# Inverse units in three products, and another order of the work within each step

## The reference

```python
def _attn_ref(x, w_r, w_i, b_r, b_i):          # x: 4 x 3008 x 256
    X = np.fft.rfft(x, axis=1)
    Xr, Xi = (X.real.astype(np.float32), X.imag.astype(np.float32))
    Yr = Xr @ w_r - Xi @ w_i + b_r
    Yi = Xr @ w_i + Xi @ w_r + b_i
    lam = 0.01
    Yr = np.sign(Yr) * np.maximum(np.abs(Yr) - lam, 0.0)
    Yi = np.sign(Yi) * np.maximum(np.abs(Yi) - lam, 0.0)
    Y = Yr.astype(np.float64) + 1j * Yi.astype(np.float64)
    return np.fft.irfft(Y, n=x.shape[1], axis=1).astype(np.float32)

def _moe_ref(x, w_in, w_out, alpha):           # 12032 x 256, 256 x 2048, 2048 x 256
    h = x @ w_in
    g = np.maximum(h, 0.0) + alpha * np.minimum(h, 0.0)
    return (g @ w_out).astype(np.float32)
```

## Time and profile before

| | us |
|---|---|
| median of three runs | 1419.74 |
| lowest, highest | 1418.84, 1421.32 |
| the profiled execution, its own time | 1419.24 |
| its span in the profile | 1417.4 |
| busy in it: TensorE, VectorE | 1380.9, 951.3 |
| busy in it: ScalarE, GpSimd | 743.6, 308.7 |

### The profile page before, as it was taken

One profiled execution on the slowest core, in us unless ns is written; L12 is line 12 of the kernel. 1 busy time (PEld: TensorE's weight loads), 2 busy tenths in 40 slices (PEclk: granted clock), 3 DMA queues, 4 the chain that ended last, 5 costly groups with the idle time before them and its releaser, 6 DMA issues. The chain is left out here.

```text
span 1417.4 us, 21513 instructions
## 1 busy us (share of the span) xinstructions
PE 1380.9 (97%) x7012; PEld 1166.2 (82%) x7012; DVE 951.3 (67%) x1826; ACT 743.6 (52%) x1646; POOL 308.7 (22%) x353
## 2 busy tenths in 40 slices
PE   6998999999999999999999999999999999999997
PEld 3987888888888888888888888888888888888886
DVE  5786677877855557877765556787876555555554
ACT  3775555656544445655654445565664444444443
POOL 1433532222201412222211231222220010001000
PEclk9999999999999999999999999999999999999999
DMA  6644522122210431212211232222121011101101
GB/s 223 193 151 133 158 61 74 52 67 64 47 39 25 134 100 53 71 48 75 56 34 39 73 109 69 58 70 63 53 53 37 16 32 26 19 14 32 21 15 15
DMA packets 163166, 94.72 MB, mean 67 GB/s; under 512 B 110424, under 2 KB 140680, under 8 KB 163056
## 3 DMA queue, kind: packets, MB, share of 16 engines
q1 hardware_dynamic: 158250, 88.91, 23.6%
q10 hardware_dynamic: 4806, 4.45, 1.0%
HBM read 55.78 MB, written 37.49 MB: 66 GB/s over the span
## 5 line engine op out<-in xcount | busy, mean ns | idle before, releaser
L1014 DVE SCALAR_TENSOR_TENSOR g_raw<-negpart,keep,h_ps 128x502 f32<-128x502 f32 (+1 forms) x384 | 282.4, 736 | 375.0 <-ACT negpart L790 372.5
L790 ACT ACTIVATE negpart<-h_ps 128x502 f32<-128x502 f32 (+1 forms) x384 | 224.7, 585 | 471.4 <-PE h_ps L464 471.2
L464 PE MATMUL out_ps<-g_hi,wout_hi 128*128 128x502 f32 (+1 forms) x768 | 313.3, 408 | 6.6 <-DVE g_lo L915 4.7
L464 PE MATMUL h_ps<-y_hi,win_hi 128*128 128x502 f32 (+1 forms) x768 | 300.6, 391 | 0.8 <-DVE y_lo L915 0.5
L464 PE MATMUL h_ps<-y_lo,win_hi 128*128 128x502 f32 (+1 forms) x768 | 300.1, 391 | 0.0
L464 PE MATMUL out_ps<-g_hi,wout_lo 128*128 128x502 f32 (+1 forms) x768 | 300.0, 391 | 0.0
L464 PE MATMUL h_ps<-y_hi,win_lo 128*128 128x502 f32 (+1 forms) x768 | 299.5, 390 | 0.0
L464 PE MATMUL out_ps<-g_lo,wout_hi 128*128 128x502 f32 (+1 forms) x768 | 299.0, 389 | 0.0
L915 DVE TENSOR_TENSOR g_lo<-g_raw,g_hi 128x502 fp32r<-128x502 f32 (+1 forms) x384 | 271.3, 707 | 0.1
L799 ACT ACTIVATE g_hi<-g_raw 128x502 fp32r<-128x502 f32 (+1 forms) x384 | 236.0, 615 | 0.3 <-DVE g_raw L1014 0.3
L464 PEld LDWEIGHTS out_ps<-g_hi,wout_hi 128*128 128x128 f32 x768 | 145.0, 189 | 39.5 <-DVE g_lo L915 10.7
(11 more groups left out here) (121 smaller groups left out, 1972.6 us busy)
## 6 DMA issues: line engine op xcount, KB each, us to landing
pair_raw<-fwd_scratch SPq DMA_DIRECT2D x96, 128.0 KB, 2.2
back_raw<-inv_scratch SPq DMA_DIRECT2D x61, 192.0 KB, 2.6
table<-in_twiddles_dram SPq DMA_DIRECT2D x28, 384.0 KB, 3.5
x_raw<-in_x_dram SPq DMA_DIRECT2D x64, 160.0 KB
inv_scratch<-inv_sb SPq DMA_DIRECT2D x36, 256.0 KB, 2.2
fwd_scratch<-staging SPq DMA_DIRECT2D x44, 192.0 KB, 2.1
out_dram<-turned SPq DMA_DIRECT2D x124, 40.0 KB, 2.0
inv_scratch<-inv_sb SPq DMA_DIRECT2D x24, 128.0 KB, 2.6
```

The lines of the kernel that those rows point to most:

```text
L464: mm = pe.matmul(ps, lhs, rhs, start=(first and n == 0), stop=(last and n == len(terms) - 1), **kw)
L790: act.activation(negpart[:, q % 2, 0:size], h_ps[:, q % 2, 0:size], ACT.Relu, scale=-1.0).then_inc(negpart_done, 1)
L1014: dve.scalar_tensor_tensor(g_raw[:, q % 2, 0:size], negpart[:, q % 2, 0:size], keep[:, m:m + 1], h_ps[:, q % 2, 0:size], ALU.mult, ALU.add ...
```

## The change

**Three matmuls.** For the pairs in the loop the load brings the first 32 of the 96 rows a second time into partitions 96 to 127 of `back_raw`, and the remaining 64 rows of each of the two blocks into the two halves of a spare buffer (`inv_sb[:, 2]`): four DMAs where there was one. ScalarE splits all 128 partitions of back_raw and then the 128x256 of the spare buffer (its hi goes for the moment into the second half of back_lo). VectorE, in the new `rest_first`, replaces partitions 96 to 127 of back_hi by the lo parts of those 32 rows. GpSimd makes the lo parts of the remaining rows for both blocks in one 128x256 operation. In `idft_parts` the rows 96 to 127 hold the hi columns of the first 32 rows again, zeros beside them. So back_hi with 188 columns gives hi x hi, hi x lo and a third of lo x hi; one more matmul with the new table `idft_rest` (188 columns: the remaining rows for block 0, then for block 1, zeros between) gives the rest for both blocks. A unit is three matmuls of 188 columns.

**Order in a step.** TensorE: output before inverse1. ScalarE: split_pair and split_back directly behind split_bent, the twiddle split there too and one step earlier, split_y near the end. VectorE: rest_pair and rest_first before shrink, rest_y last. GpSimd: twiddle rest one step earlier. y_part now lies in the buffer of bias.

```diff
         idft_parts = sb("idft_parts", [P, 2, NA], F32R)
+        idft_rest = sb("idft_rest", [P, 2, NA], F32R)
...
         shr_hi, shr_lo = (sb(f"shr_{h}", [P, 2, DIM], F32R) for h in ("hi", "lo"))
         inv_sb = sb("inv_sb", [P, 3, DIM])
 
-        back_raw = sb("back_raw", [ROWS, 2 * DIM])
+        back_raw = sb("back_raw", [P, 2 * DIM])
         back_hi, back_lo = (sb(f"back_{h}", [P, 2, 2 * DIM], F32R) for h in ("hi", "lo"))
...
 
         def back_arrived(eng, v):
             if v < HEAD_V:
                 eng.wait_ge(head_loaded[v], 16 * 6)
             else:
-                eng.wait_ge(back_loaded, 16 * (v - HEAD_V + 1))
+                eng.wait_ge(back_loaded, 64 * (v - HEAD_V + 1))
 
         def out_place(s):
             return s % OUT_HEAD if s < S_EARLY else (s - S_EARLY) % OUT_RING
...
                 if v == HEAD_V:
                     for k in range(3):
                         sp.wait_ge(inv_stored[k], 16 * GROUPS)
@@ -345,6 +351,11 @@
                     sp.wait_ge(couple_stored, 16 * PAIRS // 2 * g)
                 sp.dma_start(back_place(v).rearrange("r (b d) -> r b d", b=2),
                              inv_dram[g, :, b:b + 2, :]).then_inc(back_loaded, 16)
+                sp.dma_start(back_raw[ROWS:P, :].rearrange("r (b d) -> r b d", b=2),
+                             inv_dram[g, 0:P - ROWS, b:b + 2, :]).then_inc(back_loaded, 16)
+                for k in range(2):
+                    sp.dma_start(inv_sb[64 * k:64 * k + 64, 2, :],
+                                 inv_dram[g, P - ROWS:ROWS, b + k, :]).then_inc(back_loaded, 16)
 
             def load_head(v):
 
...
             def inverse1(u):
                 v, h = divmod(u, 2)
                 pe.wait_ge(back_lo_done, v + 1)
+                if v >= HEAD_V:
+                    pe.wait_ge(back_part_done, v - HEAD_V + 1)
                 if u == 0:
...
+                if u >= I_HEAD:
+                    for b in range(2):
+                        d = slice(b * DIM + h * P, b * DIM + (h + 1) * P)
+                        pe.matmul(i_bank(u)[:, b * 2 * NA:(b + 1) * 2 * NA], back_hi[:, v % 2, d], parts,
+                                  start=b == 0, stop=False, skip_group_check=True)
+                    pe.matmul(i_views(u)[0], back_lo[:, v % 2, h * P:(h + 1) * P], idft_rest[:, :, :],
+                              start=False, stop=True, skip_group_check=True).then_inc(back_mm, 1)
+                    return
                 for b in range(2):
                     d = slice(b * DIM + h * P, b * DIM + (h + 1) * P)
                     both = i_bank(u)[:, b * 2 * NA:(b + 1) * 2 * NA]
-                    if u < I_HEAD:
-                        hi, lo = back_hi[:, v % 2, d], back_lo[:, v % 2, d]
-                        mm = product(both[:, 0:NA], [(hi, parts[:, 0:NA]), (hi, parts[:, NA:2 * NA]),
-                                                     (lo, parts[:, 0:NA])])
-                        continue
-                    pe.matmul(both, back_hi[:, v % 2, d], parts, start=True, stop=False, skip_group_check=True)
-                    mm = pe.matmul(both[:, 0:NA], back_lo[:, v % 2, d], parts[:, 0:NA], start=False, stop=True,
-                                   skip_group_check=True)
+                    hi, lo = back_hi[:, v % 2, d], back_lo[:, v % 2, d]
+                    mm = product(both[:, 0:NA], [(hi, parts[:, 0:NA]), (hi, parts[:, NA:2 * NA]), (lo, parts[:, 0:NA])])
                 mm.then_inc(back_mm, 1)
 
...
@@ -656,12 +672,12 @@
                     p = p_unit(f, m, 0)
                     if p is not None:
                         forward2(p)
+                    q = f * STEPS + m - LAG
+                    if q >= 0:
+                        output(*divmod(q, STEPS))
                     u = i_unit(f, m)
                     if u is not None:
                         inverse1(u)
-                    q = f * STEPS + m - LAG
-                    if q >= 0:
-                        output(*divmod(q, STEPS))
                     p = p_couple(f, m, 5)
                     if p is not None:
                         inverse2(p - 1)
...
@@ -773,7 +789,11 @@
                 back_arrived(act, v)
                 if v >= 2:
                     act.wait_ge(back_mm, 2 * v - 2)
-                act.activation(back_hi[0:ROWS, v % 2, :], back_place(v), ACT.Copy).then_inc(back_hi_done, 1)
+                if v < HEAD_V:
+                    act.activation(back_hi[0:ROWS, v % 2, :], back_place(v), ACT.Copy).then_inc(back_hi_done, 1)
+                    return
+                act.activation(back_hi[:, v % 2, :], back_raw[:, :], ACT.Copy)
+                act.activation(back_lo[:, v % 2, DIM:2 * DIM], inv_sb[:, 2, :], ACT.Copy).then_inc(back_hi_done, 1)
 
             def split_y(u):
                 act.wait_ge(back_mm, u + 1)
...
-                    p = p_couple(f, m, 3)
-                    if p is not None:
-                        above_couple(p)
-                    p = p_unit(f, m, 0)
-                    if p is not None:
-                        copy_more(p)
-                    u = i_unit(f, m)
-                    if u is not None:
-                        split_y(u)
-                    p = p_couple(f, m, 3)
-                    if p is not None:
-                        split_couple(p)
-                    p = p_unit(f, m, 0)
-                    if p is not None:
-                        split_whole(p)
                     p = p_unit(f, m, -2)
                     if p is not None:
                         split_pair(p)
                     v = i_bpair(f, m - 2)
                     if v is not None:
                         split_back(v)
+                    p = p_unit(f, m, -3)
+                    if p is not None and p % 3 == 0:
+                        split_tw(p // 3)
+                    p = p_couple(f, m, 3)
+                    if p is not None:
+                        above_couple(p)
+                    p = p_unit(f, m, 0)
+                    if p is not None:
+                        copy_more(p)
+                    p = p_couple(f, m, 3)
+                    if p is not None:
+                        split_couple(p)
+                    p = p_unit(f, m, 0)
+                    if p is not None:
+                        split_whole(p)
                     if f == 0 and m % 2 == 0 and m // 2 + 2 < CHUNKS:
                         split_ffw(m // 2 + 2)
-                    p = p_unit(f, m, -2)
-                    if p is not None and p % 3 == 0:
-                        split_tw(p // 3)
                     p = p_unit(f, m, 0)
                     if p is not None:
                         split_sum(p)
                         if p % 3 == 0:
                             split_itw(p // 3)
+                    u = i_unit(f, m)
+                    if u is not None:
+                        split_y(u)
                     p = p_couple(f, m, 5)
                     if p is not None:
                         copy_couple(p)
...
-                part = y_part[:, :].rearrange("p (b a) -> p b a", b=2)
+                part = y_part.rearrange("p (b a) -> p b a", b=2)
                 dve.wait_ge(y_hi_done, u + 1)
+                if u == I_HEAD:
+                    dve.wait_ge(biased_done, PAIRS)
...
+            def rest_first(v):
+                dve.wait_ge(back_hi_done, v + 1)
+                rest(back_hi[ROWS:P, v % 2, :], back_raw[ROWS:P, :], back_hi[ROWS:P, v % 2, :]).then_inc(back_part_done, 1)
...
@@ -1118,6 +1147,12 @@
                         turn(f - 1, 1)
                     if s_unit(f, m + 2) is not None:
                         split_x(s_unit(f, m + 2), False)
+                    p = p_unit(f, m, -2)
+                    if p is not None:
+                        rest_pair(p)
+                    v = i_bpair(f, m - 2)
+                    if v is not None:
+                        rest_first(v)
                     p = p_couple(f, m, 3)
...
+                    p = p_unit(f, m, 0)
+                    if p is not None:
+                        rest_whole(p)
+                    p = p_couple(f, m, 3)
+                    if p is not None:
+                        rest_couple(p)
+                    if f == 0 and m % 2 == 0 and m // 2 + 2 < CHUNKS:
+                        rest_win(m // 2 + 2)
                     u = i_unit(f, m)
                     if u is not None:
                         rest_y(u)
-                    p = p_unit(f, m, 0)
-                    if p is not None:
-                        rest_whole(p)
-                    p = p_couple(f, m, 3)
-                    if p is not None:
-                        rest_couple(p)
-                    if f == 0 and m % 2 == 0 and m // 2 + 2 < CHUNKS:
-                        rest_win(m // 2 + 2)
-                    p = p_unit(f, m, -2)
-                    if p is not None:
-                        rest_pair(p)
...
-                rest(back_lo[0:ROWS, v % 2, :], back_place(v), back_hi[0:ROWS, v % 2, :]).then_inc(back_lo_done, 1)
```

(4 more changed lines are left out.)

37 lines of the change are left out of this document (23 added, 14 removed).

## The result

The changed kernel takes **1435.69 us** (median; 1432.69 to 1437.18) where the kernel before takes 1419.4: a ratio of 1.011, 95% interval 1.0091 to 1.0129. It is 16 us slower, and 1413.0 had been forecast. The profiled execution took 1435.66 us, 16.4 more than the one before (1419.24).

A forecast was written before the change was run, and what follows sets the result against it. TensorE's queue was taken to bound the kernel, with small waits for g_lo. From 1419.2, less 13.4 for matmuls, less 4.5 for order gains, plus 11.7 for order losses, came 1413.0 us; range 1404.5 to 1418.5.

The forecast's parts named there:

- What bounds the kernel: Whole span: TensorE, busy 97%, bounds; a change costs only where TensorE waits, in the loop chiefly for g_lo, 10.7 us.
- about 20 us for 10.7: TensorE's weight queue: a sign that waits for g_lo would grow from 10.7 to about 20 us.
- Part 1, the matmuls: TensorE's inverse units: 122 units go from four matmuls to three at 0.112 us each, 13.4 us less.
- columns rival: TensorE's units: a matmul costs its columns, 564 before and after, so no matmul gain; 1426 or 1418 us; chance 0.09.
- Part 2, new work: ScalarE, VectorE, GpSimd, loads: split 0.31 us, rest_first 0.69, GpSimd's rest 0.8; loads hidden, free in light tiles.
- late bend rival: VectorE's load steps: bend is late in every one, 24 us more, giving 1430 us; chance 0.09.
- Part 3, gains of the order: Loop cycles: earlier twiddles and pair work remove waits, 1.5 us a cycle, 4.5 us less; bounds 0 and 8.
- the longest wait: TensorE in tile 3 and its like: up to 1.1 us for pair_lo, forecast not to go but to move to g_lo.
- Part 4, losses of the order: Loop cycles: unit behind output and later bend make TensorE wait, 11.7 us more; bounds 3 and 20.
- The three places: Tile 3, steps 10 and 6, and tile 1, step 8, with repetitions: 1.5, 1.5 and 0.5 us more a cycle.
- Two more places at 0.15: Each cycle: the remaining late places beyond those worked out, two of them, losing 0.15 us each.
- VectorE also makes win_lo: Tile 0: VectorE has this extra operation there, so the new order loses 0.3 us.

The follow-up runs named there:

- products_only: The changed kernel's three products, loads and splits, with all four engine loops in the order of the kernel before; 1413.29 us, ratio 0.9947.
- rest_first_one_step_later: products_only with rest_first at the same place one step later; 1465.91 us, ratio 1.0302.
- rest_first_cut: products_only with rest_first cut to 2 of its 512 columns, leaving lo parts of 32 rows out of the result; 1411.96 us, ratio 0.9931.
- y_late_only: products_only with split_y near the end of ScalarE's step and rest_y last on VectorE; 1427.25 us, ratio 1.0033.
- only_unit_behind: products_only with the unit behind the output on TensorE; 1419.55 us, ratio 0.999.
- y_late_and_unit_behind: products_only with split_y and rest_y late and the unit behind the output; 1432.81 us, ratio 1.0073.
- unit_and_y_early: The changed kernel with the unit ahead of the output again and split_y and rest_y in their old places; 1414.65 us, ratio 0.9952.
- pair_early_only: products_only with split_pair directly behind split_bent and rest_pair ahead of shrink; 1413.79 us, ratio 0.994.

## Why the prediction was wrong

**What bounds the kernel.** Right: TensorE's queue and g_lo. Nearly all of the loss is in waits for g_lo, none in light tiles (their steps changed by 0.3 us in sum, to the better). Of the signs written down, "about 20 us for 10.7" was the one that missed: it is 40.4.

**Part 1, the matmuls: right.** Three starts 0.11 apart, 122 matmuls less, 0.33 us a unit with its effect on the hidden matmul behind. The columns rival is out: 564 columns would take what they took before. By the formula of the Trainium skill for an isolated gap (TensorE: Matmul & The Clock Gate, Back-to-back issue gap) 188 columns would take 0.08 us, an estimate; the section itself says that the formula under-counts narrow matmuls that stand among weight loads. The trace has 0.11 in this stream, so the formula can't be used for it. But "all in TensorE's queue" was only half of it. A shorter queue is a gain where TensorE decides. In the steps that VectorE decides it is handed back at once, and of the 13.4 us products_only kept 8, the new order 1 to 3.

**Part 2, new work: right.** ScalarE's split has rows of 0.40 and 0.41 us, but what it adds to the queue is the distance to the next start, and that is the 0.31 of the forecast:

```profile
336.63 0.40 ACT L796 ACTIVATE back_lo<-inv_sb 128x256 fp32r<-128x256 f32 x1
336.94 0.71 ACT L753 ACTIVATE above<-biased,low 128x512 f32<-128x512 f32 x1
```

(The ground given for it, "half", was a misreading: 0.43 for 256 columns is 0.63 of the 0.68 for 512.) GpSimd's back_lo takes 0.74 where it runs alone (49 of the 61 in rest_first_one_step_later; 0.8 was forecast), and 1.26 in most rows of the changed kernel, where it meets rest_first. rest_first takes 0.69 alone, as forecast from shr_lo, but 0.86 on average: most rows have 0.69, the longest 1.77, where it meets x_lo. Such a meeting in tile 0, timeline of GpSimd and of VectorE:

```profile
141.43 1.29 POOL L1183 TENSOR_TENSOR x_lo<-x_raw,x_hi 94x512 fp32r<-94x512 f32 x1 [1.36 <-DVE x_hi L945]
```

```profile
141.50 1.77 DVE L937 TENSOR_TENSOR back_hi<-back_raw,back_hi 32x512 fp32r<-32x512 f32 x1
```

It started 0.07 us after x_lo and ended 0.55 after it. The Trainium skill (SBUF — State Buffer, Who interferes with whom) says that one of the two holds the shared ports for its whole instruction and the other stands. This row and the g_lo of 1.32 above agree. That the loads are hidden was right. That light tiles are free was right, and so the late bend rival fell: it gave the right sign, but it wanted a late bend in every load step, and light load steps lose nothing while tile 2, step 4, without the split of a load, does.

**Part 3, gains of the order: wrong.** 4.5 us were forecast; the early pair, load and twiddle work brought nothing. In the medians it costs 1.4 in the one comparison and 2.9 in the other, neither clear of noise, and in the step losses -0.2 and 0.6. The waits named (tw_parts, pair_lo) did go. They were waits of TensorE that stood ahead of a later one, for g_lo, in the same steps, and the step's end is set by g_lo. The prediction said this of the longest wait and still booked a gain for the others. The earlier twiddles moreover lengthened a g_lo (tile 2, step 1).

**Part 4, losses of the order: right where it was worked, wrong by its count.** Tile 3, step 10 was replayed: bend 1.0 us later, TensorE 1.5 more. Here is VectorE of the changed kernel there, the answer to the earlier trace rows:

```profile
335.43 0.74 DVE L1038 SCALAR_TENSOR_TENSOR g_raw<-negpart,keep,h_ps 128x502 f32<-128x502 f32 x1 [0.91 <-ACT negpart L810]
...
336.68 0.42 DVE L937 TENSOR_TENSOR pair_lo<-pair_raw,pair_hi 128x256 fp32r<-128x256 f32 x1
337.12 0.69 DVE L937 TENSOR_TENSOR back_hi<-back_raw,back_hi 32x512 fp32r<-32x512 f32 x1
337.84 0.69 DVE L988 SCALAR_TENSOR_TENSOR shrunk<-biased,above 128x512 f32<-128x512 f32 x1
...
339.59 0.80 DVE L937 TENSOR_TENSOR spec_lo<-room,spec_hi 128x256 fp32r<-128x256 f32 x1 [0.72 <-ACT spec_hi L739]
340.32 0.95 DVE L937 TENSOR_TENSOR shr_lo<-shrunk,shr_hi 128x512 fp32r<-128x512 f32 x1
341.19 0.34 DVE L937 TENSOR_TENSOR bias<-work_ps,y_hi 128x188 f32<-128x188 f32 x1
...
341.83 0.73 DVE L1038 SCALAR_TENSOR_TENSOR g_raw<-negpart,keep,h_ps 128x502 f32<-128x502 f32 x1
```

The bend of before at the start of this step:

```profile
327.19 0.74 DVE L1014 SCALAR_TENSOR_TENSOR g_raw<-negpart,keep,h_ps 128x502 f32<-128x502 f32 x1 [0.91 <-ACT negpart L790]
```

From bend to bend 6.40 us, where this row and the earlier trace rows give 5.36: 1.04 later. TensorE's loss grew by 1.62. The pieces are those forecast: the wait for spec_hi that rest_y no longer fills (0.72), and spec_lo and shr_lo beside GpSimd (0.80 and 0.95 instead of 0.43 and 0.68). The three places came to 10.7 us for 10.5. In products_only they already lose 4.4 us more than before: that part is the new work of part 2, rest_first above all (0.9 is left in rest_first_cut), and the rest is the order.

The step that failed is the sentence "Two more places at 0.15". I looked for steps in which load, couple and unit fall together. But late y needs only a unit and a wait of VectorE for ScalarE that y had filled, as in tile 2, step 4, which has no load to split; and the unit behind the output needs only a late g_lo. Alone they cost 14.0 us (y_late_only) and 6.3 us (only_unit_behind), where the whole of part 4 was given 11.7. Tile 2, steps 6 and 10, tile 3, step 15 and tile 4, step 10 lose 3.2 us a cycle together (table) where the whole remainder was 0.3; tile 2, step 1 loses 0.7 more by another cause, the earlier twiddles (0.43 in y_late_and_unit_behind, 1.15 in unit_and_y_early). In tile 0 the mechanism "VectorE also makes win_lo" was named and given 0.3; rest_y now stands behind win_lo and the unit behind the output, and the two steps lose 1.8.

**The range.** 20 us was its upper bound for part 4 ("also the unworked load steps"), and 1419.2 - 13.4 + 20 is 1425.8. It stood in the working and was left out of the range, which ended at 1418.5. What the runs show against it, 10.7 + 12.9 + 2.0, is 25.6: it lies past even that bound. Of it 6.9 is there in products_only too, so it comes with the new work and not with the order.

**What would have shown it.** The row that speaks is in the view of waits as a wait that is *not* there: before, VectorE's waits for ScalarE were short in unit steps because y filled them. The waits of spec_lo for spec_hi were 22.4 us in 42 places before and are 38.4 in 72 in the changed kernel, those of shr_lo for shr_hi 11.3 and 17.2 us in 21. An operation that fills a wait has to be costed in every step in which it does, at its full duration.

A kernel that beats both is at hand: products_only at 1413.3 us, 0.5% below before [0.35 to 0.7%]; pair_early_only is level with it. The new products are worth taking, the new order isn't.

## What to carry to other kernels

Before an operation is moved to the end of an engine's step, look at what it filled: where the engine waits for another one in mid-step, the operation is free there and costs its duration ahead of the next critical one (0.65 us of 0.7 in tile 2, step 4). A shorter queue on the bounding engine gains only in the steps that this engine decides; count them before multiplying. And where a hand replay of one step gives a loss, replay all the kinds of steps that share its mechanism, not the ones that look the fullest.
